# Bonus sums by TensorE, state products on four array quarters, and re-timed loads in the attention stage of a fused attention and mixture-of-experts kernel

## The chip, the cores and the metric

One core of one Trainium2 chip runs the whole program. The metric is the device time of one execution in microseconds (us); the time of a kernel is the median of its runs.

## What is computed

The reference runs a gated linear attention, then a dense feed-forward layer, then a top-1 mixture of eight experts. Only the first is touched by the change, apart from one part of the logits (below). Cut to what matters:

```python
batch, n_heads, seq, head_dim = (4, 8, 768, 48)
def _attn_ref(r, k, v, w, u):
    for t in range(S):
        kt, vt, rt = (k[:, :, t], v[:, :, t], r[:, :, t])
        cur = np.einsum('bhd,bhe->bhde', u[None] * kt, vt)
        y[:, :, t] = np.einsum('bhd,bhde->bhe', rt, state + cur)
        state = w[None, :, :, None] * state + np.einsum('bhd,bhe->bhde', kt, vt)
```

then `h = x @ w_in; (h - tanh(h)) @ w_out`, and then the routing of 3072 tokens to eight experts by the cosine between their rows and `expert_emb`, and for each expert `relu(x @ w1) @ w2` times the gate. All of it is in float32.

## The kernel before, in words

The program has three blocks one after the other: attention, feed-forward, experts. Between two blocks all engines meet. The change lies in the attention block.

**Tiles.** Attention works in chunks of 128 tokens (`CH` = 6 chunks) for each of `B` = 4 batch rows, so in 24 tiles numbered n = 4c + b. A tile holds eight heads as four pairs q; the two heads of a pair lie in partitions 0 to 47 and 64 to 111. Within a chunk the recurrence is written as masked products of scaled operands: `rs` is r times powers of the decay, `ks` is k times inverse powers (made together as `rsks` on DVE, L454), their product per head is the score matrix (PE, L572), masked on DVE into `am` (L516). The output `y` of a tile is the sum of three parts on PE: the state times `rs` (L624), v times `am` (L632), and the bonus term, which is v scaled by the sum over d of r·k·u and is added by a transposing product of `bv` with the identity (L639). The state is updated by `kst` times v (PE L612 into `upd`) and two DVE instructions (L541, L545).

**The bonus sums.** POOL multiplies r by k (L330) and the product by u (L332) in the token-major layout; ACT sums each of the eight heads with a copy that accumulates (L397, eight instructions each with an accumulator read), then scales v by each sum into `bv` (L406, eight instructions).

**Pieces of the feed-forward weights.** With tiles b = 0 and 1 of a chunk comes a piece of `w_in` (`raw`). ACT copies it to a rounded high part (L390) and POOL subtracts that to get the low part (L336). With tiles b = 2 and 3 comes a piece of the transposed output weight `woT_sb`, which is only used after the last tile, in `logit_weights` (L591).

**What sets the order.** Every engine has a list of instructions that it runs strictly in the order of the program; semaphores hold an instruction until others are done. On PE the list is: the scores of tile n+1, then for tile n the state update, the state product, the product with `am`, the transposes of `bv`; the semaphore `summed` follows. On DVE: `am` of tile n, scaling of tile n+2 (`scale`, `scale_t`), the state of tile n. On ACT for tile n: the high part of a piece if there is one, the eight sums, the eight scalings, two store issues for tile n−2, and then `take`, the copy of `y` of tile n−1 out of PSUM (L375). On POOL for tile n: L330, L332 and, if b < 2, L336, which waits for the high part. SP issues all loads of tile n+4 after `summed` of tile n, on one queue. The decay powers are made at the start by scans and two reciprocals on DVE (L470 to L486) and one copy on ACT (L365). PE warms up with 12 products of the identity (`keep_warm`, L82).

The output y and the accumulator `upd` have two PSUM buffers each, and the copy of y in SBUF (`xt_sb`) has two.

Of the kernel before, what the change touches and what calls it, by code (L numbers as in the profile page):

```python
# [15 lines left out]
F32 = mybir.dt.float32  # L16
# [68 lines left out]
def build(nc, rkT, krv, w, u_row, w_in, w_out, w_outT, emb, tau, w12, x_dram, x2_dram, w12_h, w12_l, out):  # L85
    with ExitStack() as whole:
# [25 lines left out]
        with ExitStack() as ff_mem:  # L112
# [17 lines left out]
            xt_sb = sbf("xt_sb", [ROWS, 2, PAIRS, P])  # L130
            xt_stored = [ff_mem.enter_context(nc.semaphore(f"xt_stored{i}")) for i in range(2)]
            attention(nc, rkT, krv, w, u_row, w_in, w_outT, emb, tau, x_dram, load_group, xt_sb, xt_stored,
                      ident, consts, rtau, bank7, win_h, win_l, w_logit)
            turn_gates = feed_forward(nc, x2_dram, xg_sb, load_group, xg_loaded, xt_stored, ident, consts, bank7, win, w_ex, w_out, w_logit,
# [6 lines left out]
def attention(nc, rkT, krv, w, u_row, w_in, w_outT, emb, tau, x_dram, load_group, x_sb, x_stored,  # L141
              ident, consts, rtau, bank7, win_h, win_l, w_logit):
    EP = 32
    with ExitStack() as ctx:
# [10 lines left out]
        rkT_sb = sb("rkT_sb", [P, B, 2, PAIRS, P])  # L155
        krv_sb = sb("krv_sb", [P, B, 3, DM])
        k_sb, r_sb, v_sb = (krv_sb[:, :, i, :] for i in range(3))
# [4 lines left out]
        emb_n = sb("emb_n", [E, DM])  # L162
        embT = sb("embT", [P, KD, EP])
        wlT = sb("wlT", [P, PIECE])

        rsks = sb("rsks", [P, B, 2, PAIRS, P])
        rs, ks = (rsks[:, :, i, :, :] for i in range(2))
        kst = sb("kst", [P, 2, DM])
        am = sb("am", [P, 2, 2, 4 * P])
        rku = sb("rku", [P, 2, DM])  # L170
        rku_out = sb("rku_out", [P, DM])
# [7 lines left out]
        decay = sb("decay", [P, PAIRS])  # L179
        inv = sb("inv", [P, 8, PAIRS])  # L180
        zeros = sb("zeros", [P, P + 1])
        powers = sb("powers", [P, PAIRS, P + 1])
        prpk = sb("prpk", [P, 2, PAIRS, P])
        pk = prpk[:, 1, :, :]
        pkt = sb("pkt", [P, DM])
        wlast = sb("wlast", [P, PAIRS])
        u_sb = sb("u_sb", [P, DM])
        mask = sb("mask", [P, 4 * P])

        banks = [psum(f"bank{i}", [P, 512]) for i in range(7)] + [bank7]  # L190
        scores = [[banks[0], banks[1]], [banks[2], banks[3]]]
        y = [banks[4], banks[5]]
        upd = [banks[6], banks[7]]

        decay_clear = sem("decay_clear")
        powers_made = sem("powers_made")
        pr_made = sem("pr_made")
        wlast_made = sem("wlast_made")
# [40 lines left out]
        def landed(c):  # L239

            return 16 * (4 * c + 3)
# [1399 lines left out]
```

## Time and profile before

| | us |
|---|---|
| runs | 885.36, 887.75, 887.29 |
| median | 887.29 |
| the profiled execution | 886.88 |
| its span, first to last instruction | 885.1 |
| PE / DVE / ACT / POOL busy over the span | 838.1 / 567.2 / 518.8 / 308.3 |
| mean granted TensorE clock | 0.987 |

The profiled execution's own time is 886.88 us, of which 885.1 us is the span and 1.8 us lies around it. Views used: the timeline (each row: start us, duration us, engine, line, operation, output<-inputs, shapes, count, and in brackets the idle time before it and what ended it), the table by windows, the list of waits, the instructions of one line with their shortest, median and longest time, and the DMA view. "PEq", "SPq" and "ACTq" are the queues (sequencers) of those engines; PEld is the weight load of TensorE. Times are from the start of the span.

### The profile page before, as it was taken

To read this page: it belongs to the slowest core of one execution; us is meant where nothing else is said; L and a number is where in the kernel's file an instruction comes from. 1 tells how busy PE (TensorE), PEld (TensorE's weight loads), DVE (VectorE), ACT (ScalarE), POOL (GpSimd) and SP (SyncE) were. 2 spreads that over 40 slices of the span, in tenths; PEclk is the share of its full clock that TensorE was granted. 3 is DMA by queue.
4 is the path that set the end of the run, shared out by engine and by line. 5 is a ranking of instruction groups with operands and counts; after the bars stand their busy time and mean duration, and the time that the engine had idled before them with its cause. 6 is when DMAs were issued, how large, how long until landed. Compare 5 with 4: busy or idle time off the path is not lost. (4 is left out here: it accounts for less than half of the span.)

```text
span 885.1 us, 19003 instructions
## 1 busy us (share of the span) xinstructions
PE 838.1 (95%) x5366; PEld 744.0 (84%) x5367; DVE 567.2 (64%) x889; ACT 518.8 (59%) x1409; POOL 308.3 (35%) x343
## 2 busy tenths in 40 slices
PE   6888888999999999999999999999999999999995
PEld 5666665888899899899899899889989989989994
DVE  7788864999999999999999998721111121121120
ACT  5889886666876876877777766333333333233231
POOL 6776660222343334344333332122222222223211
PEclk7999999999999999999999999999999999999998
DMA  8999973112777977977886797378885666601100
GB/s 243 277 296 283 272 230 116 46 45 96 262 235 230 297 236 224 297 249 219 289 267 219 247 304 270 128 275 319 315 303 216 237 215 223 248 33 44 44 1 1
DMA packets 99193, 184.85 MB, mean 209 GB/s; under 512 B 9771, under 2 KB 24269, under 8 KB 99152
## 3 DMA queue, kind: packets, MB, share of 16 engines
q1 hardware_dynamic: 85200, 168.80, 58.4%
q0 software_dynamic: 3968, 10.82, 3.7%
q10 hardware_dynamic: 9984, 4.72, 2.0%
q8 instruction: 21, 0.34, 0.2%
q14 instruction: 20, 0.16, 0.1%
HBM read 119.81 MB, written 65.86 MB: 210 GB/s over the span
## 5 line engine op out<-in xcount | busy, mean ns | idle before, releaser
L1063 POOL TENSOR_TENSOR ew_l<-ew_raw,ew_h 128x512 fp32r<-128x512 f32 x96 | 126.5, 1325 | 215.0 <-DVE poly L1262 210.7
L980 PE MATMUL y_ps<-wout_h,g_h 128*128 128x392 f32 x384 | 132.0, 344 | 3.8 <-ACT x_sb L1173 3.4
L981 PE MATMUL y_ps<-wout_l,g_h 128*128 128x392 f32 x384 | 130.6, 340 | 0.0
L982 PE MATMUL y_ps<-wout_h,g_l 128*128 128x392 f32 x384 | 130.5, 340 | 0.0
L1415 DVE TENSOR_TENSOR ex_hT_l<-e_bank,ex_hT_h 128x512 fp32r<-128x512 f32 x62 | 40.0, 686 | 125.3 <-ACT ex_hT_h L1571 125.3
L980 PE MATMUL h_ps<-xT_h,win 128*128 (+1 forms) x288 | 113.1, 393 | 1.7 <-DVE diff L1243 1.6
L981 PE MATMUL h_ps<-xT_l,win 128*128 (+1 forms) x288 | 112.7, 391 | 0.0
L982 PE MATMUL h_ps<-xT_h,win 128*128 (+1 forms) x288 | 112.4, 390 | 0.0
L1153 ACT ACTIVATE g_h<-poly 128x512 fp32r<-128x512 f32 x96 | 61.1, 636 | 86.4 <-DVE poly L1262 86.0
L1571 ACT ACTIVATE ex_hT_h<-e_bank 128x512 fp32r<-128x512 f32 x62 | 33.7, 597 | 120.2 <-PE e_bank L1485 116.2
L1450 POOL DMA_INDIRECT out_dram<-ex_o_sb,put_i x31 | 31.0, 1000 | 204.2 <-ACT ex_o_sb L1555 204.2
L1407 DVE TENSOR_TENSOR ex_xT_l<-e_bank,ex_xT_h 128x384 fp32r<-128x384 f32 x31 | 17.3, 558 | 116.0 <-ACT ex_xT_h L1547 116.0
L1483 PE MATMUL e_bank<-w_ex,ex_hT_h 128*128 x248 | 86.0, 347 | 1.3 <-ACT ex_o_sb L1555 1.3
L1563 ACT ACTIVATE ex_hid<-e_bank 128x512 f32<-128x512 f32 x62 | 37.2, 600 | 79.2 <-PE e_bank L1485 79.2
L1484 PE MATMUL e_bank<-w_ex,ex_hT_h 128*128 x248 | 83.5, 337 | 0.0
L1485 PE MATMUL e_bank<-w_ex,ex_hT_l 128*128 x248 | 83.3, 336 | 0.0
L1262 DVE COPY_PREDICATED poly<-large,diff 128x512 f32<-128x512 uint8 x96 | 71.7, 747 | 16.8 <-DVE poly L1258 16.8
L1253 DVE TENSOR_TENSOR g_l<-poly,g_h 128x512 fp32r<-128x512 f32 x96 | 81.3, 847 | 0.8 <-ACT g_h L1153 0.8
L980 PEld LDWEIGHTS y_ps<-wout_h,g_h 128*128 128x128 f32 x384 | 72.0, 188 | 11.3 <-ACT x_sb L1173 4.6
L1483 PE MATMUL e_bank<-w_ex,ex_xT_h 128*128 x186 | 76.4, 411 | 0.7 <-DVE ex_xT_l L1407 0.5
L981 PEld LDWEIGHTS y_ps<-wout_l,g_h 128*128 128x128 f32 x384 | 72.1, 188 | 3.1
L1484 PE MATMUL e_bank<-w_ex,ex_xT_h 128*128 x186 | 73.5, 395 | 0.0
(187 smaller groups left out, 1927.7 us busy)
## 6 DMA issues: line engine op xcount, KB each, us to landing
ew_raw<-in_w SPq DMA_DIRECT2D x96, 256.0 KB, 3.2
w_h<-ew_h SPq DMA_DIRECT2D x96, 256.0 KB, 3.4
w_l<-ew_l SPq DMA_DIRECT2D x96, 256.0 KB, 2.6
w_ex<-w_h SPq DMA_DIRECT2D x14, 1536.0 KB, 11.5
w_ex<-w_l SPq DMA_DIRECT2D x14, 1536.0 KB, 15.2
krv_sb<-in_krv SPq DMA_DIRECT2D x24, 576.0 KB, 5.3
rkT_sb<-in_rkT SPq DMA_DIRECT2D x40, 192.0 KB, 4.0
x_dram<-xt_sb ACTq DMA_DIRECT2D x48, 96.0 KB, 5.3
```

Source lines behind the costliest of these rows:

```text
L980: pe.matmul(out, lh, rh, start=start, stop=False)
L981: pe.matmul(out, lh, rl, start=False, stop=False)
L982: return pe.matmul(out, ll, rh, start=False, stop=stop)
L1063: pool.tensor_tensor(ew_l[:, slot, :], raw, ew_h[:, slot, :].bitcast(F32), ALU.subtract).then_inc(ew_l_made, 1)
L1153: act.activation(g_h[:, f % RING, :], poly[:, f % RING, :], ACT.Copy).then_inc(gh_done, 1)
L1253: dve.tensor_tensor(g_l[:, f % RING, :], poly[:, f % RING, :], g_h[:, f % RING, :].bitcast(F32), ALU.subtract).then_inc(gl_done, 1)
L1262: dve.copy_predicated(poly[:, f % RING, :], large[:, f % 2, :], diff[:, f % 2, :]).then_inc(g_done, 1)
L1415: dve.tensor_tensor(hT_l[:, hf, :], hT_ps[hf][:, :], hT_h[:, hf, :].bitcast(F32), ALU.subtract).then_inc(hT_split, 1)
L1483: pe.matmul(ps, lh, w[:, slot, 0, cols], start=start, stop=False)
L1484: pe.matmul(ps, lh, w[:, slot, 1, cols], start=False, stop=False)
L1485: return pe.matmul(ps, ll, w[:, slot, 0, cols], start=False, stop=stop)
L1563: act.activation(hid[:, hf, :], h_ps[hf][:, :], ACT.Relu).then_inc(relued, 1)
```

## The change

1. **Bonus sums.** POOL multiplies r by k in the head-dimension-major layout (`rk`, one instruction of 112x512 instead of two of 128x384). PE multiplies `rk` of each pair with a two-column matrix of u (`bonus_of`, four products into `bank7`), placed after the scores of the same tile. ACT copies the 128x8 result (one instruction instead of eight with eight accumulator reads). r is no longer loaded in the token-major layout: `krv` of 1152 columns becomes `kv` of 768.
2. **Four quarters.** For odd pairs the two heads swap their partitions in k, r, w and u. The state product of a pair then takes the array quarters (row half, column half) 0-0 and 1-1 for even pairs, 1-0 and 0-1 for odd ones, and y of even and odd pairs lies in two banks. y has one buffer, and so has `upd`; `xt_sb` has four.
3. **Loads.** The transposed operands (`krT`) are loaded once `scaled` and `rk_made` of the tile four earlier are there; `kv` after `summed` as before. The pieces of `w_in` come with b = 2 and 3; ACT's high copy stands after `take`. The output weight is loaded in three transfers of 1 MB after the last tile's loads; `logit_weights` runs before the last tile.
4. **Power tables.** Six squarings, one reciprocal and seven doublings on DVE instead of scans; `keep_warm` 8 times instead of 12.

```diff
@@ SP
-                        wait(sp, summed, n - B + 1)
-                        if b < 2:
-                            wait(sp, low_made, 2 * c + b - 1)
...
+                        wait(sp, scaled, n - B + 1)
+                        wait(sp, rk_made, n - B + 1)
...
+                        wait(sp, summed, n - B + 1)
+                        sp.dma_start(kv_sb[:, b, :, :], kv[c, b]).then_inc(loaded[b], 16)
+                        if b >= 2:
+                            wait(sp, low_made, 2 * c + b - 3)
+                            sp.dma_start(raw[:, b - 2, :], w_in[c, b - 2]).then_inc(raw_loaded[b - 2], 16)
                 over(sp, CH, load)
+                for a in range(KD):
+                    sp.dma_start(woT_sb[:, a, :], w_outT[a]).then_inc(wo_loaded, 16)
@@ POOL
-                        pool.tensor_tensor(rku[:, b % 2, :], r_sb[:, b, :], k_sb[:, b, :], ALU.mult).then_inc(rk_made, 1)
-                        pool.wait_ge(rk_made, n + 1)
-                        pool.tensor_tensor(rku[:, b % 2, :], rku[:, b % 2, :], u_sb[:, :], ALU.mult).then_inc(rku_made, 1)
-                        if b < 2:
-                            wait_apart(pool, passed_low, (high_made, 2 * c + b + 1))
...
+                        pool.wait_ge(loadedT[b], turned_in(c))
+                        wait(pool, bonus_done, n - 1)
+                        pool.tensor_tensor(rk[0:ROWS, b % 2, :, :], krT_sb[0:ROWS, b, 0, :, :], krT_sb[0:ROWS, b, 1, :, :],
+                                           ALU.mult).then_inc(rk_made, 1)
+                        if b >= 2:
+                            wait_apart(pool, passed_low, (high_made, 2 * c + b - 1))
+                            pool.tensor_tensor(piece_of(c, b - 2, win_l_flat), raw[:, b - 2, :],
+                                               piece_of(c, b - 2, win_h_flat).bitcast(F32),
+                                               ALU.subtract).then_inc(low_made, 1)
@@ ACT
-                        if b < 2:
-                            wait_apart(act, passed_act, (loaded[b], landed(c)))
-                            act.activation(piece_of(c, b, win_h_flat), raw[:, b, :], ACT.Copy).then_inc(high_made, 1)
-                        act.wait_ge(rku_made, n + 1)
...
+                        act.wait_ge(bonus_done, n + 1)
                         wait(act, bv_made, n - 1)
-                        for h in range(H):
-                            head = slice(h * D, (h + 1) * D)
-                            last_sum = act.activation(rku_out[:, head], rku[:, b % 2, head], ACT.Copy,
-                                                      accum_out=bonus[:, b % 2, h:h + 1])
+                        act.activation(bonus[:, b % 2, :], bonus_ps, ACT.Copy).then_inc(bonus_taken, 1)
...
                         elif not isinstance(c, int) or last:
                             take(c - 1, B - 1)
+                        if b >= 2:
+                            wait_apart(act, passed_act, (raw_loaded[b - 2], 16 * (c + 1)))
+                            act.activation(piece_of(c, b - 2, win_h_flat), raw[:, b - 2, :], ACT.Copy).then_inc(high_made, 1)
@@ DVE
-                step(dve.reciprocal(inv[:, 0, :], decay[:, :]))
                 for i in range(6):
-                    step(dve.tensor_tensor(inv[:, i + 1, :], inv[:, i, :], inv[:, i, :], ALU.mult))
-                for q in range(PAIRS):
-                    scan = dve.tensor_tensor_scan(powers[:, q, :], decay[:, q:q + 1].to_broadcast([P, P + 1]), zeros[:, :],
-                                                  inv[:, 6, q:q + 1], ALU.mult, ALU.add)
...
-                dve.reciprocal(pk, powers[:, :, 1:P + 1]).then_inc(pk_made, 1)
+                    step(dve.tensor_tensor(decay[:, i + 1, :], decay[:, i, :], decay[:, i, :], ALU.mult))
+                step(dve.reciprocal(pkpr[:, :, P - 1:P + 1], decay[:, 6, :].unsqueeze(2).to_broadcast([P, PAIRS, 2])))
+                for i in range(7):
+                    n = 1 << i
...
+                    last = dve.tensor_tensor(runs[:, :, mid - 2:mid + 2:3, :], runs[:, :, mid - 1:mid + 1, :],
+                                             decay[:, i, :].unsqueeze(2).unsqueeze(3).to_broadcast([P, PAIRS, 2, n]),
+                                             ALU.mult)
@@ PE
+                def bonus_of(c, b):
+                    n = B * c + b
...
+                    pe.wait_ge(rk_made, n + 1)
+                    wait(pe, bonus_taken, n)
+                    for q in range(PAIRS):
+                        last = pe.matmul(bank7[:, 2 * q:2 * q + 2], rk[0:ROWS, b % 2, q, :], u_sb[0:ROWS, q, :],
+                                         start=True, stop=True)
+                    last.then_inc(bonus_done, 1)
...
-                        if is_first(c) or b < 2:
-                            wait_apart(pe, passed_pe, (scaled_t, n + 1), (state_new, n - 1))
+                        if is_first(c) or b == 0:
+                            wait_apart(pe, passed_pe, (scaled_t, n + 1), (state_new, n))
...
-                    wait_apart(pe, passed_pe, (y_taken, n - 1))
+                    wait_apart(pe, passed_pe, (y_taken, n))
...
-                            for s in range(2):
-                                rows = slice(s * HI, s * HI + D)
-                                last = pe.matmul(y[b % 2][rows, q * P:(q + 1) * P], state[rows, b, q, :],
-                                                 rs[rows, b, q, :], start=(q == 0), stop=False, skip_group_check=True)
+                            for half in range(2):
+                                r = row_of(q, half)
+                                rows = slice(r * HI, r * HI + D)
+                                last = pe.matmul(out_rows(q, slice(half * HI, half * HI + D)),
+                                                 state[rows, b, q, :], rs[rows, b, q, :],
+                                                 start=(q < 2), stop=False, skip_group_check=True)
...
                         if b + 1 < B:
                             score(c, b + 1)
+                            bonus_of(c, b + 1)
                         elif not last:
                             score(c + 1, 0)
+                            bonus_of(c + 1, 0)
+                        if last and b == B - 1:
+                            logit_weights()
                         tile(c, b, last)
```

In `diff` above `row_of(q, half)` is `half ^ (q & 1)` and `out_rows(q, rows)` is `y[rows, q % 2, q // 2 * P:(q // 2 + 1) * P]`.

The order on POOL in one pass of the chunk loop before (`rku` are the products for the bonus sums, `win<-raw,win` is the low part of a weight piece, `loaded0` to `loaded3` tell the tile's b):

```order
L330 TENSOR_TENSOR rku<-krv_sb 128x384 [waits bonus_made]
...
L332 TENSOR_TENSOR rku<-rku,u_sb 128x384 [waits rk_made]
...
L336 ISA [waits high_made]
L336 TENSOR_TENSOR win<-raw,win 128x512
L330 TENSOR_TENSOR rku<-krv_sb 128x384 [waits bonus_made,rku_made,loaded1]
```

And of the change, the same pass (`rk` is the product that PE now reads):

```order
L329 TENSOR_TENSOR rk<-krT_sb 112x512 [waits bonus_done,loadedT1]
L62 REGISTER_ALU [waits loadedT2]
L329 TENSOR_TENSOR rk<-krT_sb 112x512 [waits bonus_done]
L334 ISA [waits high_made]
L334 TENSOR_TENSOR win<-raw,win 128x512
L62 REGISTER_ALU [waits loadedT3]
L329 TENSOR_TENSOR rk<-krT_sb 112x512 [waits bonus_done]
```

The low part moved from tiles 0 and 1 to tiles 2 and 3. It stands between `rk` of tile 2 and `rk` of tile 3, and the second one between `rk` of tile 3 and `rk` of the next chunk's tile 0.

The order on ACT for tile b = 2 of the change (`bonus<-bank` is the copy of the sums, `xt_sb<-y` is `take` of the tile before, `win<-raw` is the high part that POOL's low part waits for):

```order
L389 ACTIVATE bonus<-bank 128x8 [waits bv_made,bonus_done]
L399 ACTIVATE bv<-kv_sb,bonus 128x48 [waits summed,bonus_taken,loaded2]
L399 ACTIVATE bv<-kv_sb,bonus 128x48 x7
L380 ISA [waits y_taken]
L380 DMA x_dram<-xt_sb 48x4x128
L380 ISA
L380 DMA x_dram<-xt_sb 48x4x128
L373 ACTIVATE xt_sb<-y 112x2x2x128 [waits xt_stored1,summed]
L413 ISA [waits raw_loaded0]
L413 ACTIVATE win<-raw 128x512
```

The high part moved from ahead of the tile's sums to behind `take`, which waits for `summed` of the tile before.

The order on PE for one tile of the change (`bank<-ksrs` are the scores, `bank<-u_sb,rk` is `bonus_of`, both of tile n+1; the rest is tile n, with `summed` raised by its last row):

```order
L561 MATMUL bank<-ksrs 128x128 [waits masked]
L561 MATMUL bank<-ksrs 128x128 x7
L574 MATMUL bank<-u_sb,rk 128x2 [waits bonus_taken,rk_made]
L574 MATMUL bank<-u_sb,rk 128x2 x3
L616 MATMUL upd<-kv_sb,kst 48x48 [waits scaled_t,state_added]
L616 MATMUL upd<-kv_sb,kst 48x48 x7
L62 REGISTER_ALU [waits y_taken]
L630 MATMUL y<-ksrs,state 48x128 [waits state_new]
L630 MATMUL y<-ksrs,state 48x128 x7
L635 REGISTER_ALU
L639 MATMUL y<-am,kv_sb 48x128 [waits masked]
L646 MATMUL y<-ident,bv 112x128 [waits bv_made]
```

Between the scores and the state update stands a new group that waits for POOL.

## Rows read from the trace of the kernel before

**Rows 1.** Windows table: length, PE, PEld, DVE, ACT, POOL busy, PEclk, DMA share, GB/s.
```profile
57.00:77.00 20.00, 16.59 (x264) 13.22 (x264) 15.73 (x23) 17.85 (x100) 13.33 (x11) 1.00 1.01 288
```
**Rows 2.** Waits from 0 to 140 us: total, times, longest.
```profile
POOL win L336 <- ACT win L390: 22.5, 11, 5.3
...
ACT xt_sb L375 <- DMA x_dram<-xt_sb: 12.2, 12, 2.4
DVE rsks L454 <- DMA raw<-in_w_in: 12.1, 9, 3.7
```
**Rows 3.** DMA view, 0 to 130 us, the queue of the loads: packets, MB, share.
```profile
q1 hardware_dynamic: 10816, 31.15, 82.0%
```
**Rows 4.** Timeline, marks of the stage: tiles 0 and 23, first feed-forward product.
```profile
20.81 1.10 PE L639 MATMUL bank<-ident,bv 128*112 128x128 f32 x4
...
30.14 1.22 DVE L454 TENSOR_TENSOR rsks<-rkT_sb,prpk 112x1024 f32<-112x1024 f32 x1 [3.70 <-DMA raw<-in_w_in]
...
135.26 0.65 PE L639 MATMUL bank<-ident,bv 128*112 128x128 f32 x4 [1.41 <-ACT bv L406]
...
143.34 0.50 PE L980 MATMUL h_ps<-xT_h,win 128*128 128x512 f32 x1
```
**Rows 5.** Timeline, PE in one tile, 112 to 117 us.
```profile
112.19 1.16 PE L572 MATMUL bank<-rsks 48*128 48x128 f32 x16 [0.80 <-DVE rsks L454]
...
113.28 0.56 PE L612 MATMUL bank<-krv_sb,kst 128*48 128x48 f32 x16
...
113.78 1.08 PE L624 MATMUL bank<-rsks,state 48*48 48x128 f32 x16
...
114.85 1.08 PE L632 MATMUL bank<-am,krv_sb 128*48 128x128 f32 x16
...
115.86 0.65 PE L639 MATMUL bank<-ident,bv 128*112 128x128 f32 x4
```
**Rows 6.** Timeline, PE's warm-up by whole-array products, 2 to 8 us.
```profile
2.15 5.51 PE L82 MATMUL bank<-ident 128*128 128x128 f32 x24 [2.15 <-POOL ident L312]
```
**Rows 7.** Timeline, take, high part and low part, and what follows on POOL.
```profile
115.58 0.60 ACT L375 ACTIVATE xt_sb<-bank 112x512 f32<-112x512 f32 x1 [0.83 <-DMA x_dram<-xt_sb]
...
116.07 0.62 ACT L390 ACTIVATE win<-raw 128x512 fp32r<-128x512 f32 x1
...
116.87 1.44 POOL L336 TENSOR_TENSOR win<-raw,win 128x512 fp32r<-128x512 f32 x1 [3.48 <-ACT win L390]
...
121.62 1.27 POOL L336 TENSOR_TENSOR win<-raw,win 128x512 fp32r<-128x512 f32 x1 [1.16 <-ACT win L390]
...
122.84 1.01 POOL L330 TENSOR_TENSOR rku<-krv_sb 128x384 f32<-128x384 f32 x1
```
**Rows 8.** Line L336: count, shortest, median and longest ns, first and last start.
```profile
L336 POOL TENSOR_TENSOR win<-raw,win x12: 1263/1360/2330, 13.2 to 121.6; 128x512 f32 x8, 128x512 fp32r<-128x512 f32 x4
```
**Rows 9.** Timeline, DVE and POOL side by side, 69 to 72 us.
```profile
69.56 1.23 DVE L454 TENSOR_TENSOR rsks<-rkT_sb,prpk 112x1024 f32<-112x1024 f32 x1 [0.85 <-DMA raw<-in_w_in]
69.60 2.52 POOL L330 TENSOR_TENSOR rku<-krv_sb 128x384 f32<-128x384 f32 x1 [1.21 <-DMA raw<-in_w_in]
```
**Rows 10.** Timeline, the power tables on DVE.
```profile
3.37 1.14 DVE L472 TENSOR_TENSOR inv<-inv 128x4 f32<-128x4 f32 x6
...
6.32 3.35 DVE L482 RECIPROCAL prpk<-powers 128x512 f32<-128x512 f32 x1
```
**Rows 11.** Windows table, columns as in Rows 1, around an idle stretch of PE.
```profile
30.00:31.40 1.40, 0.00 (x0) 0.00 (x0) 1.25 (x2) 1.40 (x7) 1.12 (x1) 1.00 1.09 328
31.40:33.00 1.60, 1.58 (x20) 1.35 (x22) 1.60 (x4) 0.08 (x1) 1.52 (x2) 0.72 1.07 372
33.00:35.00 2.00, 2.00 (x30) 1.98 (x32) 0.69 (x2) 1.33 (x5) 0.77 (x1) 0.50 1.02 226
35.00:37.00 2.00, 2.00 (x26) 1.43 (x22) 1.93 (x7) 1.97 (x17) 1.90 (x1) 0.87 1.02 357
```
**Rows 12.** Timeline, the logit weights on PE.
```profile
135.84 2.78 PE L591 MATMUL bank<-woT_sb,embT 128*32 128x512 f32 x24
```

More of the change, by code:

```diff
@@ L138, in build, with attention @@
                 first_loaded, turn_gates)
-def attention(nc, rkT, krv, w, u_row, w_in, w_outT, emb, tau, x_dram, load_group, x_sb, x_stored,
+def attention(nc, krT, kv, w, u_cols, w_in, w_outT, emb, tau, x_dram, load_group, x_sb, x_stored,
               ident, consts, rtau, bank7, win_h, win_l, w_logit):
@@ L213, in attention @@
         emb_clear = sem("emb_clear")
+        wo_loaded = sem("wo_loaded")
         wl_done = sem("wl_done")
@@ L422, in _ @@
                 store(CH - 1, B - 1)
-                act.wait_ge(wl_done, 1)
-                act.activation(wlT[:, :], upd[0][:, :], ACT.Copy).then_inc(wl_taken, 1)
                 act.wait_ge(wl_turned, 1)
@@ L536, in chunk @@
                         if is_first(c):
-                            dve.tensor_tensor(state[0:ROWS, b, :, :], by_pair(upd[b % 2]), wide(wlast),
+                            dve.tensor_tensor(state[0:ROWS, b, :, :], by_pair(upd), wide(wlast),
                                               ALU.mult).then_inc(state_new, 1)
@@ L629, in tile @@
                     for q in range(PAIRS):
-                        for s in range(2):
-                            head = slice((2 * q + s) * D, (2 * q + s + 1) * D)
-                            last = pe.matmul(y[b % 2][s * HI:s * HI + D, q * P:(q + 1) * P], v_sb[:, b, head],
-                                             am[:, b % 2, s, q * P:(q + 1) * P],
-                                             start=(is_first(c) and q == 0), stop=False,
+                        for half in range(2):
+                            r = row_of(q, half)
+                            last = pe.matmul(out_rows(q, slice(half * HI, half * HI + D)), v_sb[:, b, head_at(q, r)],
+                                             am[:, b % 2, r, q * P:(q + 1) * P],
+                                             start=(is_first(c) and q < 2), stop=False,
                                              skip_group_check=True)
@@ L1582, with swapped @@
     from concourse.bass_utils import run_bass_kernel_spmd as _run
+    def swapped(x):
+        x = x.copy()
+        x[:, 1::2] = x[:, 1::2, ::-1].copy()
+        return x
     def by_d(*xs):
@@ L1592, in by_token, with in_columns @@
     def by_token(x):
-        x = x.reshape(B, H, CH, P, D)
+        x = swapped(x.reshape(B, PAIRS, 2, CH, P, D)).reshape(B, H, CH, P, D)
         return np.ascontiguousarray(x.transpose(2, 0, 3, 1, 4)).reshape(CH, B, P, DM)
     def pairs(x):
-        return np.ascontiguousarray(x.reshape(PAIRS, 2, D).transpose(1, 2, 0))
+        return np.ascontiguousarray(swapped(x.reshape(1, PAIRS, 2, D))[0].transpose(1, 2, 0))
+    def in_columns(x):
+        cols = np.zeros((2, HI, PAIRS, 2), np.float32)
+        for r, rows in enumerate(pairs(x)):
+            cols[r, 0:D, :, r] = rows
+        return np.ascontiguousarray(cols.reshape(2 * HI, PAIRS, 2)[0:ROWS])
     def by_piece(x):
```

231 lines of the change are left out of this document (112 added, 119 removed).

## The prediction

> **What bounds the kernel now.** I read the table by windows first, then the waits, then the timeline. In attention DMA is busy the whole time (share 1.01 at 288 GB/s) while PE has 16.6 of 20 us, DVE 15.7, ACT 17.9 and POOL 13.3 [rows 1]. The waits say the same: DVE's scaling waits 12.1 us in 9 places for the last load of a tile, and `take` waits 12.2 us for a free half of `xt_sb` [rows 2]. One tile's loads and stores are 458 + 590 + 262 + 197 KB = 1.51 MB, at 292 GB/s (31.15 MB in 82% of 130 us [rows 3]) 5.2 us. The transposes of tile 0 start at 20.81 and those of tile 23 at 135.26 [rows 4]: 114.4 us for 23 tiles, 4.98 each. So the stage is held by its loads. PE alone would do a tile faster: with no wait, 1.09 us from scores to state update, 0.50 to the state product, 1.07 to the product with `am`, 1.01 to the transposes, and 0.65 for these: 4.32 us [rows 5]. After attention nothing is changed but the way in, so what follows the first feed-forward product at 143.34 [rows 4] is taken as it stands.
>
> **The change part by part.** The sum runs from the start to that product, in four stretches.
>
> *Start, −5.7 us.* Before, six squarings, scans and a reciprocal of 3.35 us end the tables at 9.7 us. The squarings stay (1.14 us); I put the small reciprocal and seven doublings of 8 to 512 columns at 2.4 us, from 0.19 us for a small step up to 0.7 us for the largest, so that the tables are there at about 7 us instead of 9.7 [rows 10]. Tile 1's transposed operands then are only 1.31 MB down the queue instead of 2.8, since the token-major r is gone, the piece of `w_in` comes later and u is tiny: at 270 GB/s that is 5.5 us less. The two gains overlap; the later of them decides, and I take 15.1 for the start of tile 0's transposes instead of 20.81. Bounds: −3 (DVE's gain alone) and −8 (both).
>
> *The 23 tiles without new waits, −12.0 us.* The load falls to 458 + 393 + 131 + 197 KB = 1.18 MB a tile, 4.0 us at the same rate, and the stall of 3.70 us at tile 4 [rows 4] goes, as its transposed operands are asked for early. PE becomes the bound. Its list gains `bonus_of`: four products with a 112x128 stationary operand and two moving columns. No row shows this. From below, the eight small products of the state update start the next group 0.50 us later [rows 5]; from above, 12 whole-array products took 5.51 us at the start [rows 6], and if that was the low clock all through, four at the high one are 0.9 us. It is a full-array group between two split ones, so nearer the second: 0.75. The state product with four quarters: at worst 1.07 as now, at best the 0.5 of a half; I take 0.70, since the weight loads don't get shorter. A tile is then 4.32 + 0.75 − 0.37 = 4.70. Over 23 tiles 108.1; less 0.70 in tiles 1 to 3 of the first chunk (no state product), 0.50 in each of the last four (no state update) and 1.85 in the last (no scores, no bonus), plus 0.3 for the turning of the embedding: 102.4 against 114.4. Bounds from the two pairs of prices: 4.45 and 5.2 a tile, −18 and −1. DVE, at 15.7 us for four tiles [rows 1], ACT, which loses eight sums and their reads, and the loads stay under 4.7. The Trainium skill (TensorEngine Tiling (Array Packing), Key Properties) says that tiles work in parallel but that a change of tiling mode drains the engine, which speaks for the whole 0.5 of gain and for another drain at `bonus_of`; by it a tile would come out near 4.6 to 4.8 as well.
>
> The single `upd` asks for DVE's sum of tile n−1 before the update of tile n; DVE has done this 2 us earlier. The single y asks for `take` of tile n−1; that needs 0.7 us after `summed`, and PE has scores, bonus and update first, 2.3 us. Both cost nothing as long as ACT is free when `summed` comes. Four buffers of `xt_sb` end the 12.2 us of waits of `take`, which were beside the loads.
>
> *The new wait, +33.6 us.* This is the term that decides. POOL's low part waits for ACT's high part, and ACT's high part now stands behind `take` of the tile before, so behind `summed`. POOL runs in order, and `rk` of the next tile stands behind the low part. PE wants it for `bonus_of` 1.09 us after `summed`, ahead of the update, state product and everything else of its tile. From the end of tile n−1's transposes: `take` starts 0.05 later, the high part 0.49 after that, POOL's low part 0.80 after the start of the high part, and the next POOL instruction 1.22 after the low part's start [rows 7]. `rk` is 512 columns, as is the low part, whose shortest is 1.26 us and median 1.36 [rows 8]; I take 1.27, and 0.1 for the hand-over to PE. Besides, POOL and DVE hold each other up where both read two operands from SBUF: a POOL product of 384 columns lasts 2.52 us beside two DVE ones, and 1.01 alone [rows 9, 7]; DVE's scaling of tile n+2 lies there until about 1.6 us after `summed`, which puts the low part back by 0.2. Sum: 0.05 + 0.49 + 0.80 + 0.20 + 1.22 + 1.27 + 0.10 = 4.13, against 1.09: 3.05 us of waiting. The Trainium skill states the sharing of the SBUF interfaces (GPSIMD Engine Reference, Specifications); the trace agrees, 2.52 against 1.01 us. The wait falls on the bonus of tile b = 3 and of the next chunk's b = 0: two a chunk, eleven in all, since the last low part has no tile behind it. Nothing hides it: PE has no other work in its list. 11 x 3.05 = 33.6. Bounds: 2.7 each (no meeting with DVE, quick hand-overs), 30; and 4.1 each, if `rk` and the low part both meet DVE, 45.
>
> *The clock, +7.2 us.* After PE sat idle for 3.3 us up to 31.42 us the granted clock read 0.72, 0.50 and 0.87 in the next 5.6 us, 1.2 instead of 2.4 GHz for part of it [rows 11]: 0.28 x 1.6 + 0.50 x 2 + 0.13 x 2 = 1.7 us of full-clock work lost; since waits lie among it I take 1.3. Where PE is idle in short pieces, 3.4 of 20 us in all, it stays at 1.00 [rows 1]. The new waits of 3.05 us lie just under the long one and far over these; I count half of the eleven. Bounds: none, and 11 x 1.7 = 19.
>
> *The way out, +0.8 us.* `logit_weights` (2.78 us [rows 12]) goes from behind tile 23 to ahead of it, so on the path in both; behind tile 23 its copy out of PSUM and the wait for it vanish too, and 8.08 us from the last transposes to the feed-forward [rows 4] become about 4.9: −3.2. In the loop it costs 2.8, and its weight may be late: behind the last tile's `kv` and piece come 3.1 MB, with the stores 4.4 MB, 15.1 us at 292 GB/s and some 2 us of issue and latency from `summed` of tile 19; PE is there after 4.4 + 4.1 + 7.2 = 15.7. Wait 1.2. Sum −3.2 + 2.8 + 1.2.
>
> **Sum:** −5.7 − 12.0 + 33.6 + 7.2 + 0.8 = +23.9 on the profiled execution's 886.88 us: 910.8. Its time stands 0.4 under the median of the three runs, so 911.
>
> **The rivals.**
> *(A) The clock falls at every wait.* The Trainium skill (TensorE: Matmul & The Clock Gate, Why this matters for your kernels) warns of a throughput drop after long idle gaps between bursts of matmuls. Here each wait would be followed by a cold stretch at up to 1.7 us, +12 over my sum: 923. For it: the one row after a long idle. Against it: my waits are shorter than that one.
> *(B) The waits are there but the clock holds and the tile is as short as its lower bound.* 911 − 7.2 − 6 = 898. For it: the short idle pieces of [rows 1] did nothing to the clock, and three of the prices were taken from the upper half.
> *(C) No wait: faster.* If the high part were done before `summed`, the low part would sit in POOL's idle time and `bonus_of` would find its operand. The sum is then −5.7 − 12.0 − 3.2 + 2.8 and up to 4 for the output weight, which PE would reach earlier: 873. It decides where the chain above takes under 1.1 us; the high and low part alone take 0.62 and 1.26. For it stands only that POOL waited 22.5 us for the high part before [rows 2] and nobody on PE waited for POOL; but then only ACT's sums read POOL's product.
> *(D) The quarters don't do what they say.* The state product stays at 1.07: +0.37 x 20 = 7, 918.
>
> **How the numbers follow.** My sum 0.45, A 0.17, B 0.17, D 0.12, C 0.07, and 0.02 that it ends level by errors in several terms. B to A give 898 to 923; with the bounds of the tile and the wait around them I say 894 to 925. A difference under 0.3%, 2.7 us, is about what a measurement of this kernel can tell from none. Faster 0.07, same 0.02, slower 0.91.
>
> **What would show it.** In the profile after: PE's `bonus_of` group waits for POOL's `rk` (L329) eleven times at about 3 us, 30 us or more in all; POOL's low part (L334) waits for ACT's high part (L413), and that begins within 1.3 us of `summed`; per chunk two tiles of about 7.7 us and two of 4.7; the DMA share in attention falls to some 0.6 to 0.8; the first transposes start at 15 us; the first feed-forward product starts near 167 us instead of 143. I am wrong if the list of waits has no entry of `bonus_of` for POOL, if the wait is under 1.5 us, or if the feed-forward and expert blocks change their length.

## The result, and the profile after

The changed kernel takes **940.27 us** against 886.33 us (884.97 to 887.75) for the kernel before on the same chip: ratio 1.060, 95% interval 1.056 to 1.064. The 940.27 is the median of 937.12, 938.96, 941.57 and a fourth run of 1353.7 us at a mean granted clock of 0.585, which isn't compared; without it the median is 938.96, so differences taken below from 940.3 can be 1.3 us too large. The direction was forecast; the size, +24 us, was not: some +54 came, and the time lies over the range of 894 to 925.

The profiled execution took 941.57 us, 54.7 more than the one of before. The marks of [rows 4] divide this up. From the list of TensorE's groups, with L639 of before now at L646 and L980 at L993:

```profile
19.44 1.10 PE L646 MATMUL y<-ident,bv 128*112 128x128 f32 x4
...
182.56 2.91 PE L591 MATMUL upd<-woT_sb,embT 128*32 128x512 f32 x24
...
187.00 0.65 PE L646 MATMUL y<-ident,bv 128*112 128x128 f32 x4
...
191.99 0.49 PE L993 MATMUL h_ps<-xT_h,win 128*128 128x512 f32 x1
```

| stretch, us | before | after | difference |
|---|---|---|---|
| start to the transposes of tile 0 | 20.81 | 19.44 | −1.4 |
| tile 0 to tile 23 | 114.45 | 167.56 | +53.1 |
| to the first feed-forward product | 8.08 | 4.99 | −3.1 |
| the rest of the execution | 743.54 | 749.58 | +6.0 |

So nearly all of it is in the 23 tiles. The list of waits from 0 to 220 us, which answers to [rows 2] (total, times, longest):

```profile
POOL win L334 <- ACT win L413: 126.1, 12, 15.0
DVE kst L455 <- PE upd L616: 74.3, 20, 6.8
ACT bonus L389 <- PE bank L574: 73.0, 24, 5.4
...
PEld bank L574 <- POOL rk L329: 31.5, 11, 3.1
PE bank L574 <- POOL rk L329: 29.4, 11, 2.9
```

The waits of `take` for a free `xt_sb` are gone, and those of DVE's scaling for its loads but for one of 0.9 us. In their place stands the last line: `bonus_of` waits for POOL's `rk` eleven times, 29.4 us in all. The first line is the head of the chain that the forecast named, POOL's low part waiting for ACT's high part; POOL's idle time costs something only because `rk` stands behind it. The second and third are engines that wait for PE, so they cost nothing by themselves. TensorE's timeline over one chunk shows a tile without a wait, and then two with one (each float32 product shows as two records, so the four of `bonus_of` are x8):

```profile
80.47 0.65 PE L646 MATMUL y<-ident,bv 128*112 128x128 f32 x4
81.05 1.16 PE L561 MATMUL bank<-ksrs 48*128 48x128 f32 x16
82.14 1.05 PE L574 MATMUL bank<-u_sb,rk 112*128 112x2 f32 x8
83.13 0.56 PE L616 MATMUL upd<-kv_sb,kst 128*48 128x48 f32 x16
83.62 0.65 PE L630 MATMUL y<-ksrs,state 48*48 48x128 f32 x16
84.21 1.08 PE L639 MATMUL y<-am,kv_sb 128*48 128x128 f32 x16
85.22 0.65 PE L646 MATMUL y<-ident,bv 128*112 128x128 f32 x4
85.80 1.16 PE L561 MATMUL bank<-ksrs 48*128 48x128 f32 x16
89.84 1.11 PE L574 MATMUL bank<-u_sb,rk 112*128 112x2 f32 x8 [2.88 <-POOL rk L329]
90.88 0.88 PE L616 MATMUL upd<-kv_sb,kst 128*48 128x48 f32 x16
91.69 1.10 PE L630 MATMUL y<-ksrs,state 48*48 48x128 f32 x16
92.73 1.74 PE L639 MATMUL y<-am,kv_sb 128*48 128x128 f32 x16
94.40 0.65 PE L646 MATMUL y<-ident,bv 128*112 128x128 f32 x4
...
99.03 1.05 PE L574 MATMUL bank<-u_sb,rk 112*128 112x2 f32 x8 [2.88 <-POOL rk L329]
...
101.17 1.95 PE L639 MATMUL y<-am,kv_sb 128*48 128x128 f32 x16
103.05 1.10 PE L646 MATMUL y<-ident,bv 128*112 128x128 f32 x4
```

From transposes to transposes the tile without a wait takes 4.75 us. The next takes 9.18, where 4.75 + 2.88 would be 7.63. The same 16 records of L639 last 1.08 us in the first and 1.74 and 1.95 in the others: the time beyond the wait is the low clock, and it falls not in the wait but on the work behind it. The chain that makes the wait is on ACT and POOL, each from its own timeline:

```profile
85.91 0.60 ACT L373 ACTIVATE xt_sb<-y 112x512 f32<-112x512 f32 x1 [0.50 <-PE y L646]
86.40 0.62 ACT L413 ACTIVATE win<-raw 128x512 f32 x1
```
```profile
87.31 1.26 POOL L334 TENSOR_TENSOR win<-raw,win 128x512 f32 x1 [14.99 <-ACT win L413]
88.53 1.26 POOL L329 TENSOR_TENSOR rk<-krT_sb 112x512 f32<-112x512 f32 x1
```

`take`, high part, low part, `rk`, product: from 85.80 to 89.84 is 4.04 us, forecast 4.13. Windows of 16 tiles (PE, PEld, DVE, ACT, POOL busy, clock, DMA share, GB/s) for the steady part of the stage:

```profile
54.80:173.50 118.70, 96.97 (x1189) 80.61 (x1188) 56.81 (x93) 46.67 (x167) 29.79 (x24) 0.80 0.54 154
```

DMA fell from a share of 1.01 at 288 GB/s [rows 1] to 0.54 at 154, so the stage is no longer load bound, and the granted clock from 1.00 to 0.80.

### The profile page after: what moved, and what is told of

Same layout as the page of the kernel before. It is cut to its first block and busy times, and to the rows that moved or that the text cites. A ratio compares the mean times of both kernels' runs of the same rounds, so it can differ in the third digit from the quotient of the medians.

```text
span 939.6 us, 18988 instructions
## 1 busy us (share of the span) xinstructions
PE 886.1 (94%) x5550; PEld 788.1 (84%) x5551; DVE 552.1 (59%) x888; ACT 480.1 (51%) x1048; POOL 270.3 (29%) x319
## 3 DMA queue, kind: packets, MB, share of 16 engines
q1 hardware_dynamic: 83888, 163.89, 53.1%
## 5 line engine op out<-in xcount | busy, mean ns | idle before, releaser
L993 PE MATMUL y_ps<-wout_h,g_h 128*128 128x392 f32 x384 | 132.1, 344 | 4.0 <-ACT x_sb L1186 3.6
L993 PE MATMUL h_ps<-xT_h,win 128*128 (+1 forms) x288 | 113.0, 393 | 1.6 <-DVE diff L1259 1.6
L993 PEld LDWEIGHTS y_ps<-wout_h,g_h 128*128 128x128 f32 x384 | 72.0, 188 | 11.5 <-ACT x_sb L1186 4.4
```

Of the source, the lines that this page charges most:

```text
L993: pe.matmul(out, lh, rh, start=start, stop=False)
```

## The experiments

Times are medians. "Marks" are the starts of tile 0's and tile 23's transposes and of the first feed-forward product.

**e1_low_behind**: the changed kernel, with POOL's low part placed behind `rk` of the next tile.

```diff
-                        if b >= 2:
-                            wait_apart(pool, passed_low, (high_made, 2 * c + b - 1))
-                            pool.tensor_tensor(piece_of(c, b - 2, win_l_flat), raw[:, b - 2, :],
...
+                        if b == 3:
+                            low(c, 0)
+                        if b == 0 and not is_first(c):
+                            low(c - 1, 1)
+                    if last:
+                        low(c, 1)
+                def low(c, i):
+                    wait_apart(pool, passed_low, (high_made, 2 * c + i + 1))
+                    pool.tensor_tensor(piece_of(c, i, win_l_flat), raw[:, i, :],
...
```

> POOL's low part of a weight piece is put behind rk of the next tile, nothing else. Theory 1 (POOL's order makes the waits, and the waits let the clock fall): no wait of bonus_of for POOL over 0.3 us, the clock at 1.00 in attention after some 30 us, tiles of 4.75 us; 23 tiles take 105 to 112 us instead of 167.9 and the kernel 877 to 887 us. Theory 2 (the clock is low because the bonus products keep the array little used, waits or not): the waits go, 32 us less, but the clock stays at 0.7 to 0.8 and the kernel takes 900 to 912. Theory 3 (the wait only moves, to rk behind the low part of the piece before): waits of 1 to 3 us are left and the kernel stays over 920.

Measured: 879.51 us against 886.40, ratio 0.993 (0.989 to 0.997). `bonus_of` doesn't wait for POOL any more, and every tile of the steady part takes 4.75 us. The window of the same 16 tiles:

```profile
41.44:116.64 75.20, 75.20 (x1190) 63.51 (x1188) 65.10 (x93) 46.67 (x167) 36.37 (x24) 1.00 0.85 237
```

PE is busy all of it, at 1.00, and 75.20 us take the place of 118.70. One instruction's place on POOL is worth some 60 us of the whole time, and without it the change is faster than before. Marks 19.30, 128.66, 133.64. The output weight is late at the end, from PE's timeline:

```profile
124.35 2.78 PE L598 MATMUL upd<-woT_sb,embT 128*32 128x512 f32 x24 [2.81 <-DMA woT_sb<-in_w_outT]
```

**e2_high_first**: ACT's high part at the head of its tile, ahead of the copy of the sums; POOL's order as in the change.

```diff
@@ ACT
+                        if b >= 2:
+                            wait_apart(act, passed_act, (raw_loaded[b - 2], 16 * (c + 1)))
+                            act.activation(piece_of(c, b - 2, win_h_flat), raw[:, b - 2, :], ACT.Copy).then_inc(high_made, 1)
                         act.wait_ge(bonus_done, n + 1)
...
-                        if b >= 2:
-                            wait_apart(act, passed_act, (raw_loaded[b - 2], 16 * (c + 1)))
-                            act.activation(piece_of(c, b - 2, win_h_flat), raw[:, b - 2, :], ACT.Copy).then_inc(high_made, 1)
```

> ACT's high part is put at the head of tiles 2 and 3, ahead of the copy of the sums, so that it no longer stands behind take; POOL's order stays. Theory 1 says that the cause is the chain summed, take, high part, low part, rk: it is cut at its other end, and the time is that of e1 within 5 us, 877 to 890. If the cause were POOL's own load (low part and rk in one tile), the waits would stay at 1 us or more and the time over 895.

Measured: 880.08 us (877.62 to 887.55), ratio 0.993 (0.990 to 0.996). No wait for POOL either. Loosening the chain at its other end gives the same, so it is the chain from `summed` through the high part that held `rk`, and not POOL's load.

**e3_fill**: the changed kernel, its order kept; while PE would wait, it multiplies the identity eleven times into free columns of `bank7`.

```diff
+                def filler(pe, n):
+                    wait(pe, bonus_taken, n)
+                    for _ in range(11):
+                        pe.matmul(bank7[:, 256:256 + P], ident[:, :], ident[:, :], start=True, stop=True)
...
+                            if b + 1 == 3:
+                                filler(pe, B * c + b + 1)
                             bonus_of(c, b + 1)
...
+                            filler(pe, B * c + B)
                             bonus_of(c + 1, 0)
```

> The changed kernel with eleven extra 128x128 products of the identity (into unused columns of bank7) ahead of bonus_of where it waits, so that PE works through the wait. If the low clock comes from PE standing idle there, the clock rises to 1.00 behind tile 3 and the kernel gets faster in spite of more work: by 15 to 28 us, to 912 to 925. If the clock is set by something else (the bonus products, or the start), it stays near 0.95 over the kernel and the time is 940 to 955.

Measured: 910.15 us (909.09 to 920.05), ratio 1.030 (1.022 to 1.037). The chain is untouched and PE gets no useful work, yet **30 us of the 61 are gone**. PE's timeline and the window of 16 tiles:

```profile
83.81 1.16 PE L561 MATMUL bank<-ksrs 48*128 48x128 f32 x16
84.90 2.72 PE L569 MATMUL bank<-ident 128*128 128x128 f32 x22
87.87 1.05 PE L579 MATMUL bank<-u_sb,rk 112*128 112x2 f32 x8 [0.25 <-POOL rk L329]
88.86 0.56 PE L621 MATMUL upd<-kv_sb,kst 128*48 128x48 f32 x16
...
90.95 0.65 PE L651 MATMUL y<-ident,bv 128*112 128x128 f32 x4
```
```profile
50.56:149.57 99.01, 96.98 (x1365) 83.76 (x1364) 57.74 (x93) 46.68 (x167) 29.85 (x24) 1.00 0.64 181
```

The tile with a wait is now 7.72 us, 4.75 and the wait of 2.97, which makes 32.7 for eleven; the whole kernels differ by 910.2 − 879.5 = 30.6, as only e1 has the output weight late, by 2.8. The low clock is the rest, 940.3 − 910.2 = 30.1 us, but not all of it lies behind the waits. In the profiled executions tile 0 to tile 23 took 167.56 and 142.25 us: 25.3 less, of which 2.3 are in the first tile, before any wait (7.36 and 5.05 us). So 23 us lie behind the waits, 2.1 each, and 2.5 each in the window of 16 tiles with eight waits, (118.70 − 99.01) / 8. Another 5.5 us lie behind the first feed-forward product, where no run ties them to the waits.

**e9_fill5**: e3 with five products for eleven.

```diff
-                    for _ in range(11):
+                    for _ in range(5):
```

> As e3, but with five extra products at each of the eleven waits instead of eleven, so that PE still stands idle for some 1.7 us of each (2.8 us in the changed kernel, under 0.6 us in e3). If only the long idle pieces let the clock fall, the clock stays up and the time is e3's, 908 to 913. If the clock follows the share of idle time, it still falls behind part of the waits and the time lies between, 915 to 930.

Measured: 923.32 us (919.91 to 926.61), ratio 1.042 (1.038 to 1.046). Some of the waits were followed by the low clock and some not: behind one of 1.60 us at 55.15 every group kept its short duration, and behind the one of 1.58 us shown here none did. The waits (total, times, longest), one tile, and the window:

```profile
PE bank L579 <- POOL rk L329: 14.0, 10, 1.8
```
```profile
81.62 1.36 PE L579 MATMUL bank<-u_sb,rk 112*128 112x2 f32 x8 [1.58 <-POOL rk L329]
82.91 0.89 PE L621 MATMUL upd<-kv_sb,kst 128*48 128x48 f32 x16
...
84.76 1.95 PE L644 MATMUL y<-am,kv_sb 128*48 128x128 f32 x16
```
```profile
55.00:165.00 110.00, 100.75 (x1245) 84.63 (x1247) 55.41 (x90) 46.17 (x167) 27.39 (x23) 0.83 0.59 174
```

PE is busy 92% of this window and the clock reads 0.83, while before it was busy 83% of [rows 1] at 1.00: the share of idle time alone doesn't decide. Nor does the length of one idle piece, for in the kernel before a longer one, 1.84 us, left the clock high:

```profile
97.31 1.16 PE L572 MATMUL bank<-rsks 48*128 48x128 f32 x16 [1.84 <-DVE rsks L454]
...
101.35 0.65 PE L639 MATMUL bank<-ident,bv 128*112 128x128 f32 x4
```

What decides between the two cases was not found.

**e4_warm20**: the changed kernel with `keep_warm` 20 times instead of 8.

```diff
-                keep_warm(pe, banks[0], ident, 8)
+                keep_warm(pe, banks[0], ident, 20)
```

> keep_warm 20 times at the start instead of 8, so that PE works until about 9 us. If the low clock of the first 28 us comes from the shortened warm-up and the idle time behind it (5.7 to 9.3 us), the first tiles run at the high clock and the kernel gets 5 to 9 us faster, 931 to 935. If the clock would be low there anyhow, it is the same or up to 1 us slower.

Measured: 938.09 us (934.59 to 938.28), ratio 1.057 (1.052 to 1.062). Little came back, 2.2 us or, without the run of 1353.7, 0.9. The tiles ahead of the first wait now ran at the high clock but for the end of tile 0, and the waits then brought the low one (tile 1's transposes last 0.65 us at 22.91, tile 2's 1.10 at 30.82). The loss sits behind the waits, not in the warm-up.

**e5_no_swap**: e1 with the row half equal to the column half, so two quarters instead of four; y stays in two banks.

```diff
-            return half ^ (q & 1)
+            return half
...
-        x[:, 1::2] = x[:, 1::2, ::-1].copy()
```

> The kernel of e1 with the swap of the odd pairs undone (row half = column half for every pair; y still in two banks). If four quarters are what brings the state product from a pitch of 1.07 us to 0.58, it goes back to 1.07, a tile takes 5.2 us instead of 4.75 and the kernel 20 x 0.49 = 10 us more than e1, 889. If it is the two banks of y that do it, the pitch stays at 0.58 and the time at 879.

Measured: 885.16 us, ratio 0.998 (0.996 to 1.001), 5.6 us over e1. PE's timeline, where the next group starts 1.01 us after the state product instead of 0.58:

```profile
61.11 1.08 PE L637 MATMUL y<-ksrs,state 48*48 48x128 f32 x16
62.12 1.08 PE L646 MATMUL y<-am,kv_sb 128*48 128x128 f32 x16
```

The quarters do what they say, 0.42 us a tile. In 20 tiles this is 8.4 us; 2.8 of them don't show in the time, since in e5 the later stage no longer waits for the output weight as e1 does. Of the 6.9 us that e1 gains over the kernel before, the quarters bring most.

**e8_bonus_one**: e1 with one of the four bonus products. It leaves out the bonus sums of six of the eight heads.

```diff
-                    for q in range(PAIRS):
+                    for q in [0]:
                         last = pe.matmul(bank7[:, 2 * q:2 * q + 2], rk[0:ROWS, b % 2, q, :], u_sb[0:ROWS, q, :],
```

> The kernel of e1 with only one of the four bonus products of a tile (the other six heads get a stale bonus sum). bonus_of took 0.99 us of a tile on PE where I had put 0.75. If its price is in the number of weight loads, it falls to about 0.3 us and a tile to 4.0 to 4.1 us if nothing else binds, 15 us less. If a tile stays at 4.3 or more, DVE (3.9 to 4.2 us of work a tile) or DMA is the next bound behind PE.

Measured, in one execution: 867.27 us. From the start of the group to the next falls from 0.98 to 0.32 us, and a tile from 4.75 to between 4.1 and 4.5.

```profile
50.00:100.00 50.00, 48.41 (x823) 39.10 (x812) 49.59 (x71) 34.79 (x124) 31.68 (x19) 1.00 0.97 262
```

So a two-column product costs PE about 0.22 us ((0.98 − 0.32) / 3). With less of it DVE becomes the bound, 49.59 of 50 us, and the loads stand close behind at 0.97. `bonus_of` whole is 0.98 of PE's 4.75 us.

**e6_wo_early**: e1 with the output weight's three transfers between the last chunk's loads. For this the last pass of the load loop is written out, and its transposed operands come in two transfers a tile instead of one.

```diff
+                        if last and b > 0:
+                            sp.dma_start(woT_sb[:, b - 1, :], w_outT[b - 1]).then_inc(wo_loaded, 16)
-                for a in range(KD):
-                    sp.dma_start(woT_sb[:, a, :], w_outT[a]).then_inc(wo_loaded, 16)
```

> The kernel of e1 with the three 1 MB transfers of the output weight issued between the loads of the last four tiles instead of behind them. In e1 logit_weights waited 2.8 us for them. If DMA has room (share 0.86 in attention), that wait goes and the kernel gains 2 to 3 us, 876 to 878. If the transfers get in the way of the last tiles' loads, PE waits there instead, and it is the same or slower.

Measured: 879.51 us (875.52 to 883.69), ratio 0.989 (0.985 to 0.994). The wait of 2.81 us is gone. Its gain doesn't show in the median, for the start of this kernel has two courses:

```profile
10.00:20.00 10.00, 10.00 (x81) 9.14 (x80) 7.99 (x11) 4.18 (x18) 4.93 (x3) 0.50 1.03 274
20.00:30.00 10.00, 10.00 (x80) 8.47 (x78) 4.23 (x6) 3.80 (x12) 0.77 (x1) 0.50 0.46 130
```

In the profiled execution (883.69) PE ran without a pause at a clock of 0.50 until 36 us, and tiles 0 and 2 had their transposes at 19.44 and 34.16; in e1's at 19.30 and 27.93.

**e7_low_behind_warm20**: e1 with the edit of e4.

```diff
-                keep_warm(pe, banks[0], ident, 8)
+                keep_warm(pe, banks[0], ident, 20)
```

> The kernel of e1 with keep_warm 20 times. In e1 the first tile ran at the low clock, and in the profiled run of e2 the first two. If PE's idle time before 9 us does this, the transposes of tile 1 start at 23 us instead of 24 to 27 in every run: 1 to 3 us faster, 876 to 879, with a narrower spread than e1's 877 to 884. Otherwise the same as e1.

Measured: 877.87 us, ratio 0.986 (0.981 to 0.991), but its runs lie in two groups, 875.1 to 877.9 and 885.0 to 888.7. The profiled one (885.0) had the high clock in tile 0's scores, then an idle piece of PE of 1.44 us while tile 1's operands were loaded, and from there the low clock until about 38 us: a longer warm-up doesn't settle the course of the start. The median over e1 is not told apart.

**e10_before_wo_last**: the kernel before, with its pieces of the output weight loaded behind all tiles.

```diff
-                        else:
-                            sp.dma_start(piece_of(c, b, woT_flat), w_outT[c, b - 2]).then_inc(loaded[b], 16)
...
                 over(sp, CH, load)
+                for c in range(CH):
+                    for i in range(2):
+                        sp.dma_start(piece_of(c, i, woT_flat), w_outT[c, i]).then_inc(wo_loaded, 16)
```

> The kernel before with one part of the change alone: the twelve pieces of the output weight are loaded behind all tiles' loads. If the tiles before are held by their loads, 1.38 MB a tile instead of 1.51 shorten a tile from 4.98 to some 4.7 us, and the last transposes come 5 to 7 us earlier, of which a late output weight gives 0 to 3 back: 881 to 885. If they are held by an engine, the first to last transposes stay at 114 us and the time at 886 or more.

Measured: 887.27 us against 884.93, ratio 1.003 (1.001 to 1.006). In the stage it did gain: tile 0 to tile 23 took 110.2 us instead of 114.45. The DMA share stayed at 0.98, and `bv` of ACT became the next wait on PE (of the waits, 0 to 140 us):

```profile
PEld bank L640 <- ACT bv L408: 10.9, 10, 2.4
DVE rsks L456 <- DMA raw<-in_w_in: 10.5, 7, 3.2
```

The 4.2 us, and 1.1 of an earlier start, were given back in the profiled execution: 1.3 between the last transposes and the first feed-forward product (9.33 us instead of 8.08), and 4.1 behind it, 745.9 us to the end of the span instead of 741.8. The median of eight runs shows no gain either. By itself, then, moving the weight brings nothing to the old kernel; why the part behind the stage took longer was not found.

**e11_wo_early_warm20**: e6 with the edit of e4.

```diff
-                keep_warm(pe, banks[0], ident, 8)
+                keep_warm(pe, banks[0], ident, 20)
```

> The kernel of e6 with keep_warm 20 times: the fastest version so far, in more runs. 875 to 878 where the clock rises by 20 us, 883 to 885 where it rises only after 30 us; if the longer warm-up does nothing to that, both are seen again.

Measured: **874.47 us** (873.41 to 879.27) against 884.93, ratio 0.989 (0.986 to 0.992), the fastest here of those that compute everything: 66 us under the change as made. Marks 20.28, 126.55, 131.63.

## Why the prediction was right or wrong

**The clock: the step that failed.** The forecast had the right mechanism and mis-sized this term: it priced one cold stretch at 1.3 us from [rows 11], counted half of the eleven waits, +7.2, and held 19 for the bound. Filling the waits gave back 30.1 us of the whole, 25.3 of it in the stage and 23 of that behind the waits, 2.1 each; the low clock came behind all eleven. The profiled execution came 30.8 us over the forecast's 910.8: 20.4 in the stage, of which the clock is 25.3 − 7.2 = 18.1, then 4.3 at the start and 6.0 behind the stage. Two things were misjudged. First the condition: idle of 3.3 us was taken as the known case and 3.05 as doubtful, since short pieces did nothing in [rows 1]. The rows of before left open all that lies between, and e9 shows the clock falling behind some pieces of 1.58 us. Second the size: in [rows 11] the clock had recovered after about 5 us, with more idle among it; here it dropped later, on the dense part of the tile, and ten of the eleven tiles with a wait still had it at their transposes (1.03 to 1.10 us, 0.65 otherwise). The Trainium skill (TensorE: Matmul & The Clock Gate, HAM oscillation — how this bites in real kernels) describes a loop whose wait throttles the clock again in every pass. The trace agrees, with the low clock behind each of eleven waits at 2.1 us apiece. The waits of the Trainium skill's loop are longer, some 3 to 5 us (same section); here 2.1 to 2.9 us were enough. This was rival A, which the forecast gave 0.17 and priced by the same row, 923 at most. Its mechanism is what happened, and its price of 1.7 us a wait was too low.

**The wait: right.** Eleven waits of up to 2.9 us, 29.4 in the list, 32.7 by the steady tiles of e3, against 33.6. The chain is 4.04 us against 4.13. The 0.2 for a meeting of POOL and DVE didn't come: `rk` and the low part took 1.26 us each, as alone. The Trainium skill's shared SBUF interfaces (GPSIMD Engine Reference, Specifications), which the forecast put into that term, thus played no part at this place, although the rows of before show them [rows 9], and so does the changed kernel's start, where `rk` of tile 1 took 2.31 us beside DVE's scaling.

**The tile: right, by luck.** 4.75 us against 4.70, by three errors that nearly cancel: the state product 0.58 instead of 0.70, the transposes 0.58 to the next group instead of 0.65, `bonus_of` 0.98 instead of 0.75. The bound of 4.45 doesn't follow from the forecast's own lower prices, 0.50 for each of the two groups, which give 4.25. Rival D, quarters without effect, fell by e5.

**The start: mis-sized.** −5.7 forecast, −1.4 to −1.5 measured (19.44, and 19.30 in e1). The seven doublings took 3.46 us against 2.4 for them and the reciprocal together, and once the load no longer held it, the way to tile 0's transposes was PE at the low clock. From DVE's timeline of the changed kernel, and then PE's of e1:

```profile
4.53 3.46 DVE L471 TENSOR_TENSOR pkpr<-pkpr,decay 128x8 f32<-128x8 f32 x7
```
```profile
9.17 2.08 PE L568 MATMUL bank<-ksrs 48*128 48x128 f32 x16
11.18 1.87 PE L581 MATMUL bank<-u_sb,rk 112*128 112x2 f32 x8
```

Scores of 1.16 us last 2.08 there, the bonus of 1.05 us 1.87. The forecast moved the old start forward by what the loads gain and never asked how long PE's own list takes from the tables on: 10.1 us from 9.17 to 19.30.

**The way out: right.** 4.98 us against 4.9 from the last transposes on. The output weight was 2.81 us late in e1, against 1.2 (the forecast's own 15.1 + 2 − 15.7 gives 1.4); in the change itself it wasn't late at all, as the stage was so slow.

**The sum without waits.** By the forecast's terms −5.7 − 12.0 + 0.8 = −16.9; e1 measured −6.9. Of the 10 missing, 4.2 are the start. First to last transposes is 109.4 instead of 106.4 (102.4 and the logit weights with their wait), 3.0, of which 1.6 is the later output weight. Another 1.4 came behind the first feed-forward product, and 1.4 is the profiled execution against the medians.

**The rest of the execution** was to stay, and took 6.0 us more in the profiled one. It is where the routing hands over to the experts. The same stretch, 407 to 444 us behind the first feed-forward product, in the windows of the changed kernel and of the one before:

```profile
598.99:635.99 37.00, 35.27 (x181) 31.43 (x180) 18.60 (x48) 10.11 (x25) 7.12 (x11) 0.77 0.39 121
```
```profile
550.34:587.34 37.00, 34.55 (x204) 29.93 (x203) 20.21 (x51) 12.32 (x29) 7.09 (x11) 0.95 0.46 148
```

From the last feed-forward group to the transposes behind the first expert's products (L1512 before, L1528 after) takes 28.3 us before and 34.0 after, 5.7 of the 6.0; the same twelve records (L840, L853) last 1.5 and 2.75 us, so it is the low clock again. Among the eleven experiments (e10 aside) the code there is the same, and before and after differ there only in buffers and waits for stores; yet from the first feed-forward product to the end of the span the eleven experiments took 741.9 to 745.9 us, one trace each, with the 745.9 in e10, where the stage is nearly the old one. The changed kernel's 747.6 lies above all of them. Whether its slow stage has a part in it was not shown, and what decides it is open.

**Rival B**, the waits with the clock held, comes close to e3, and that took 910.2: its 898 needed the lower bound of the tile and the earlier start as well, and neither came.

**Rival C**, no wait and 873, is what the kernel becomes once the chain is cut: 879.5 in e1 and 874.5 with the edits of e4 and e6 on top (e11). The point from which it decides, a chain under 1.1 us, was far off in the change as made.

## What to carry to other kernels

Before a helper's work is placed on an engine that runs in order, ask which result for the critical engine stands behind it, and what the helper itself waits for: a low part that nobody needs for many us, in front of an operand that is needed in 1.1 us, cost some 60 us here. Price an idle piece on TensorE as the wait plus the clock behind it, here 2.1 to 2.5 us on top of a wait of up to 2.9, and give that term a wide range where the rows of before have no idle piece of its length. If a wait can't be removed, filling it with idle products gave the clock's part back here; filling less than half of it gave back part. After a bound has been lifted, add up the next engine's own list from the start, at the clock that it has there.

## What the runs showed that was not expected

- The clock falls behind some idle pieces of 1.6 us in tiles of 7.7 (e9), and not behind others of the same length, nor behind one of 1.84 us in the kernel before or those of [rows 1], though these are a larger share.
- In the start PE can be busy 10.00 of 10 us at a clock of 0.50 for over 15 us (the changed kernel from 10 to 28 us, e6 to 36, e7 from 16 to about 38), while other executions of nearly the same program rise at about 20 us (e1, e3, e8). It is worth about 7 us of the stage: e6's first feed-forward product starts at 138.09 and e1's at 133.64, though e6 has 2.8 us of wait less. More warm-up alone doesn't decide it (e7), and its cause wasn't found.
- The clock column and the durations can disagree: e1 reads 1.00 for 10 to 20 us, where the scores last 2.08 us and tile 0's transposes 1.10, as at the low clock. The durations decide.

```profile
10.00:20.00 10.00, 10.00 (x80) 9.13 (x78) 7.92 (x11) 4.18 (x18) 4.84 (x3) 1.00 1.04 269
```

- A product of a 112x128 stationary operand with only two moving columns takes 0.22 to 0.25 us, as long as the filler of e3 with 128 columns (eleven in 2.72 us, 0.25 each).
